# Attention, expert network and feed-forward network on one core: a reordered start, smaller weight transfers and an earlier seam

## The chip, the cores and the metric

The kernel runs on one core of a Trainium2 chip. A core has TensorE (PE, matrix products), VectorE (DVE), ScalarE (ACT), GpSimd (POOL) and SyncE (SP, which here only issues DMAs). PE writes to eight banks of PSUM; everything else lives in SBUF. The metric is the time of the device for one execution, in microseconds (us), lower is better; three executions were timed and one more was profiled.

## The reference, cut to what matters

```python
# 1. gated linear attention, B=4, H=8, S=768, D=48
for t in range(S):
    state = alpha[:, :, t, :, None] * state + einsum('bhd,bhe->bhde', k[:, :, t], v[:, :, t])
    y[:, :, t] = einsum('bhd,bhde->bhe', q[:, :, t], state)
x = y as 3072 rows of 384
# 2. first network: each row goes to the one expert (of 8) with the largest cosine
expert_idx = argmax(xn @ en.T / tau, axis=1); gate_w = its softmax probability
for e in range(E):
    h = maximum(x[mask] @ w1[e], 0)              # 384 -> 1024
    out[mask] = gate_w[mask, None] * (h @ w2[e]) # 1024 -> 384
# 3. second network, the same weights for all rows
h = x @ w_in                                     # 384 -> 2048
return maximum(0.01 * h, h) @ w_out              # 2048 -> 384
```

## The kernel before

**Stages.** The attention fills the first 120 us or so, and the routing (which row goes to which expert, a table of slots) the next 15. The first network then runs to about 441 us and the second to the end. All products have float32 operands cut into a high part (rounded by ACT to fp32r) and a low part (the rest, by DVE), and PE makes three products for each: high by high, high by low, low by high (`PARTS`). So each operand needs an ACT pass and then a DVE pass: `gx_round`/`gx_rest` for the gathered rows, `h_round`/`h_rest` for the hidden values, `split_hi`/`split_lo` for the weights, `y_round`/`y_rest` for the rows of the second network.

**First network.** Rows are sorted by expert into 31 blocks (`WINDOWS`) of 128 slots; block w uses buffers w & 1. POOL gathers a block's rows into `xg`; PE turns them (`turn_gx`, line 1484); ACT and DVE make `gxT`; PE computes the hidden values in two halves of 9 products (`block_hidden`, line 1508); ACT applies relu. Then the hidden values must be turned as well. For odd blocks, block 0 and block 30 PE does it (`turn_h`, line 1519) and `h_round` reads PSUM (line 815). For the other even blocks (`by_squares`) DVE turns 32 by 32 squares and SP moves the squares by 16 small DMAs (`hds<-hs`), and `h_round` reads those (line 819). DVE makes the low part (lines 1255 and 1258), and PE sums the second product over 24 products (`contract`, line 1528). DVE copies the sums to `ys` (line 1302), POOL scatters them to `y_rows`, which is in memory.

Each engine runs a `step(w, u)` for every block, in order of program, and its instructions wait on semaphores. In step w, PE does the hidden part of block w + 2, turns the rows of block w + 3, and then contracts block w. ACT does, in this order: `h_round(w)`, `relu(w + 2)` twice, `gx_round(w + 3)`, and where the block table says that a new expert follows (`follower`), `first_weights` for W1 or `second_weights` for W2. DVE has the matching order: `h_rest(w)`, its turn of block w + 2, `gx_rest(w + 3)`, small work, splits, copy of the sums. Only block 0's steps hold extra work: block 1's hidden part, the rows of block 2 turned after `turn_h(0, 0)`, and `place_slots`, 13 short DVE instructions (lines 1185 to 1212) that make `slot_dst`, the row to which each slot is scattered.

**Weights.** There are ten sets: eight experts, then `SET_IN` and `SET_OUT`, the second network's. A set has two halves (W1 and W2) of 12 KB a partition, 1536 KB in all. Memory delivers a half to `raw`; ACT writes the high part in three pieces, DVE the low part in three, into the set of `wts` with that parity. After DVE has read a half of `raw`, the next one may be loaded, and `load_half` is called right behind `split_hi` by the same engine, so ACT waits there for DVE (`w_lo`), then issues the DMA. ACT issues 16 of these, SP the first two (expert 1) and, before those, six smaller ones of 512 KB for expert 0 (`load_first`, line 489).

```python
def second_weights(w, e):
    act.wait_ge(ye_ready, w + 1)
    split_hi(act, e, next_set(act, e), W2_PIECES)
    load_half(act, 1, next_expert(act, e))
```

**Second network.** Six groups of 512 rows. For each of 16 slices of 128 hidden features, PE computes `inner` (9 products, line 1555) into one of two banks; ACT scales by 0.01 (`small`, line 909), DVE takes the maximum (`g`, line 1316), ACT and DVE make the parts of `gs` (912, 1318), and PE adds to the sums of four tiles (`outward`, line 1602, 12 products). `inner` runs two slices ahead. The first two slices of group 0 are computed in step 30, ahead of block 30's `contract`; before that, rows of group 0 are turned in step 29 (`y_turn`, `y_round`, `y_rest`). PE waits for `ys_ready` of block 30 before it goes on, since bank 6 is shared.

Of the kernel before, what the change touches and what calls it, by code (L numbers as in the profile page):

```python
# [24 lines left out]
def build(nc, qka, v, emb, tau, weights, x_dram, y_dram, gate_dram, out):  # L25
# [14 lines left out]
    WINDOWS = N // P + E - 1  # L40
# [34 lines left out]
    with ExitStack() as ctx:  # L75
# [328 lines left out]
        def split_hi(act, n, par, pieces):  # L404
            for j in pieces:
                if j % 3 == 0:
                    act.wait_ge(raw_in[j // 3], n * 16 + 48)
                cols = slice(j * PC, (j + 1) * PC)
                act.activation(set_of(par, 0, cols), raw[:, cols], ACT.Copy).then_inc(w_hi[j // 3], 1)  # L409

# [7 lines left out]
        def load_half(eng, half, n):  # L418

            eng.wait_ge(w_lo[half], n * 3)  # L420
            at = slice(half * 3 * PC, (half + 1) * 3 * PC)
            src = weights[n, half] if isinstance(n, int) else weights[ds(n, 1), half].rearrange("a p n -> (a p) n")
            eng.dma_start(raw[:, at], src, max_dma_last_dim=2048).then_inc(raw_in[half], 16)

        W1_PIECES, W2_PIECES = range(0, 3), range(3, 6)

# [279 lines left out]
        def _(act):  # L706
# [89 lines left out]
            def gx_round(w, u):  # L796
                act.wait_ge(gx_turned, w + 1)
                act.activation(gxT[:, u, 0], gxps, ACT.Copy).then_inc(gx_hi, 1)
# [41 lines left out]
            relu(0, 0, 1)  # L840
            act.wait_ge(tables_ready, 2)

            def y_round(t, u, k):
                act.wait_ge(yt_turned, t * KD + k + 1)
                act.activation(yT[:, 1 - u, 0, k], yf[:, (u * KD + k) % 2], ACT.Copy).then_inc(yt_hi, 1)

            def step(w, u):
                if isinstance(w, int) and w == 0:
                    for half in range(2):
                        relu(1, 1, half)  # L850
                    e, first = follower(act, 1)
                    with act.If(first > 0):
                        first_weights(0, 1)
                        first_weights(1, e)
                for half in range(2):
                    h_round(w, u, half)
                if isinstance(w, int) and w == 0:
                    gx_round(2, 0)
                    with act.If(act.snap(E - first) > 0):
                        first_weights(0, 1)  # L860
                if ahead(w, 2):
                    for half in range(2):
                        relu(w + 2, u, half)
                if ahead(w, 3):
                    gx_round(w + 3, 1 - u)
                if ahead(w, 2):
                    e, first = follower(act, w + 2)
                    with act.If(first > 0):
                        first_weights(w + 2, e)
                e, first = follower(act, w)  # L870
                with act.If(first > 0):
                    second_weights(w, e)
                if isinstance(w, int) and w == 1:
                    act.wait_ge(shift_done, 1)
                    act.activation(ex[:, :, :], lg[:, :, :], ACT.Exp).then_inc(exp_done, 1)
                if isinstance(w, int) and w == WINDOWS - 2:
                    for k in range(KD):
                        y_round(0, 0, k)
                if not ahead(w, 1):
                    split_hi(act, SET_OUT, 1, W1_PIECES)  # L880

            each_window(act, step)
# [19 lines left out]
            def groups(i, last):  # L902
                for u in range(2):
                    t = i * 2 + u
                    for f in range(FT):
                        s = t * FT + f
                        act.wait_ge(g_ready, s + 1)
                        act.wait_ge(g_done, s + 1)
                        act.activation(small[:, f % 2], gps[f % 2][:, :], ACT.Copy, scale=0.01).then_inc(small_done, 1)  # L909
                        act.wait_ge(g_done, s + 3)  # L910
                        act.wait_ge(l2_done, s + 1)
                        act.activation(gs[:, f % 4, 0], g[:, f % 2], ACT.Copy).then_inc(g_hi, 1)  # L912
                        if Y_FROM < f <= Y_FROM + KD and not (last and u == 1):
                            y_round(t + 1, 1 - u, f - Y_FROM - 1)
                        if f == 1 and t > 0:
                            for tt in range(TG):
                                o_copy(t - 1, 1 - u, tt)
                        if t == 0 and 2 <= f < 2 + len(W2_PIECES):
                            act.wait_ge(ye_ready, WINDOWS + 1)
                            split_hi(act, SET_OUT, 1, W2_PIECES[f - 2:f - 1])  # L920
# [7 lines left out]
        def _(dve):  # L928
# [237 lines left out]
            def y_turn(t, u, k):  # L1166

                if k == 0:
# [2 lines left out]
                dve.transpose(yf[:, (u * KD + k) % 2].rearrange("p (n r) -> p n r", r=SQ),  # L1171
                              yl[:, u, :, k * SQ:(k + 1) * SQ]).then_inc(yt_turned, 1)

            def y_rest(t, u, k):
                dve.wait_ge(yt_hi, t * KD + k + 1)
                dve.tensor_tensor(yT[:, 1 - u, 1, k], yf[:, (u * KD + k) % 2], yT[:, 1 - u, 0, k].bitcast(F32),
                                  ALU.subtract).then_inc(yt_lo, 1)
# [83 lines left out]
            def step(w, u):  # L1261
                if isinstance(w, int) and w == 0:
                    e, first = follower(dve, 1)
                    with dve.If(first > 0):
                        split_lo(dve, 1, 1, W1_PIECES)
                        split_lo(dve, e, next_set(dve, e), W1_PIECES)
                for half in range(2):
                    h_rest(w, u, half)
                if isinstance(w, int) and w == 0:
                    gx_rest(2, 0)  # L1270
                    with dve.If(dve.snap(E - first) > 0):
                        split_lo(dve, 1, 1, W1_PIECES)
                if ahead(w, 2) and by_squares(w + 2, u):
                    turn_h(w + 2, u)
                if ahead(w, 3):
                    gx_rest(w + 3, 1 - u)
                if isinstance(w, int) and w == 0:
                    place_slots()
                if isinstance(w, int) and w == 1:
                    shift_logits()  # L1280
                if isinstance(w, int) and w == 2:
                    make_gates()
                if ahead(w, 2):
                    e, first = follower(dve, w + 2)
                    with dve.If(first > 0):
                        split_lo(dve, e, next_set(dve, e), W1_PIECES)
                e, first = follower(dve, w)
                with dve.If(first > 0):
                    split_lo(dve, e, next_set(dve, e), W2_PIECES)
                if isinstance(w, int) and w == WINDOWS - 2:  # L1290
                    y_turn(0, 0, 0)
                    y_turn(0, 0, 1)
                    y_rest(0, 0, 0)
                    dve.wait_ge(yt_lo, 1)
                    y_turn(0, 0, 2)
                    y_rest(0, 0, 1)
                    y_rest(0, 0, 2)
                if not ahead(w, 1):
                    split_lo(dve, SET_OUT, 1, W1_PIECES)
                wait_scattered(dve, w, u, dve_turns)  # L1300
                dve.wait_ge(ye_ready, w + 2)
                dve.tensor_copy(ys[:, u, 0:D], yeps).then_inc(ys_ready, 1)  # L1302
# [1 line left out]
            each_window(dve, step, apart=2)  # L1304


            dve.sem_inc(g_done, 2)

            def groups(i, last):
                for u in range(2):  # L1310
                    t = i * 2 + u
                    for f in range(FT):
                        s = t * FT + f
                        dve.wait_ge(small_done, s + 1)

                        dve.tensor_tensor(g[:, f % 2], gps[f % 2][:, :], small[:, f % 2], ALU.max).then_inc(g_done, 1)  # L1316
                        dve.wait_ge(g_hi, s + 1)
                        dve.tensor_tensor(gs[:, f % 4, 1], g[:, f % 2], gs[:, f % 4, 0].bitcast(F32),  # L1318
                                          ALU.subtract).then_inc(g_lo, 1)
# [12 lines left out]
        def _(pe):  # L1332

            pe.sem_inc(ye_ready, 1)
            pe.sem_inc(l2_done, 4)
            pe.wait_ge(consts_made, MADE)

            def keep_busy(n, to, left, right):
# [232 lines left out]

            def step(w, u):
                if isinstance(w, int) and w == 0:
                    block_hidden(1, 1)
                if isinstance(w, int) and w == 0:
                    turn_h(0, 0)
                    turn_gx(2, 0)
                if ahead(w, 2):
                    block_hidden(w + 2, u, (lambda: turn_h(w, u)) if u == 1 else None)
                elif not by_squares(w, u):  # L1580
                    turn_h(w, u)
                if ahead(w, 3):
                    turn_gx(w + 3, 1 - u)
                if not ahead(w, 1):
                    pe.wait_ge(w_lo[0], SET_IN * 3 + 3)
                    pe.wait_ge(relu_done, WINDOWS * 2)
                    for f in range(2):
                        inner(0, 0, f)
                e = pe.snap(table(pe, w) & (E - 1))
                par = pe.snap(e & 1)  # L1590
                pe.wait_ge(w_lo[1], e * 3 + 3)
# [106 lines left out]
```

## Time and the profile before

| what | value |
|---|---|
| median of 3 runs | 845.28 us (842.88 to 846.42) |
| profiled execution | 847.34 us |
| its span, first to last instruction | 845.3 us |
| mean granted clock of PE | 0.992 |
| PE busy | 820.9 us, 97% |
| DVE, ACT, POOL busy | 434.2, 343.0, 203.4 us |

A busy share is of the span. PE takes a product of 128x512 in 0.23 us at full clock; its busy time is no proof of its peak rate. Where PE stands idle, the view of waits names the instruction that ended the idle time.

### The profile page before, as it was taken

How to read it: one execution, taken by the hardware profiler on the slowest of the kernel's cores; microseconds unless marked ns; L12 is line 12 of the kernel's file. 1: busy time of each engine (PE TensorE's matmuls, PEld its weight loads, DVE VectorE, ACT ScalarE, POOL GpSimd, SP SyncE). 2: the span in 40 equal slices, each digit the busy share in tenths (PEclk: the TensorE clock that was granted, in tenths of full speed). 3: DMA queues.
4: the chain of work that ended last, by engine and by line, in shares of the span. 5: the costliest groups of instructions: out<-in, count | busy, mean ns of one | idle time of the engine just before them, and what ended most of it. 6: DMA issues, size and time to landing. Idle time of an engine off the chain costs nothing.

```text
span 845.3 us, 17159 instructions
## 1 busy us (share of the span) xinstructions
PE 820.9 (97%) x5379; PEld 736.8 (87%) x5380; DVE 434.2 (51%) x672; ACT 343.0 (41%) x643; POOL 203.4 (24%) x279
## 2 busy tenths in 40 slices
PE   7999999799999999999989999999999999999998
PEld 7888887689889999889979998998998998998997
DVE  6899986664455465464355533533533433443332
ACT  3455564444444444453334323323323333333233
POOL 5666622033233223332214003003003001000100
PEclk8999999999999999999999999999999999999999
DMA  9987664545564447667113201201011000000101
GB/s 229 256 247 233 209 216 140 159 152 163 179 211 146 147 143 180 224 202 182 52 4 41 38 1 38 38 1 38 14 24 37 0 0 28 10 1 0 38 1 38
DMA packets 61719, 85.81 MB, mean 102 GB/s; under 512 B 26279, under 2 KB 40147, under 8 KB 61680
## 3 DMA queue, kind: packets, MB, share of 16 engines
q1 hardware_dynamic: 39952, 45.24, 20.1%
q10 hardware_dynamic: 15840, 25.23, 9.5%
q0 software_dynamic: 5888, 14.85, 5.2%
q8 instruction: 22, 0.36, 0.2%
q14 instruction: 17, 0.14, 0.1%
HBM read 63.69 MB, written 15.64 MB: 94 GB/s over the span
## 4 chain that ended last, share of the span: by engine, by line
PE 85%; DVE 5%; issue 3%; ACT 2%; ACTq 1%; DMA 1%; POOL 1%; DVEq 1%; SPq 0%; POOLq 0%
PE bank L1555 24%; PE bank L1602 24%; PE bank L1528 12%; PE bank L1508 12%; PE bank L1350 3%; PE bank L1390 2%; PE bank L1367 2%; DVE wts L415 1%; PE bank L1519 1%; PE bank L1356 1%; PE bank L1398 1%; ACT wts L409 1%; PE bank L1410 1%; DMA qkas<-qka 1%; ACTq L385 1%
## 5 line engine op out<-in xcount | busy, mean ns | idle before, releaser
L1555 PE MATMUL bank<-yT,wts 128*128 128x512 f32 x864 | 217.1, 395 | 1.6 <-DVE g L1316 1.6
L1602 PE MATMUL bank<-wts,gs 128*128 128x384 f32 x1152 | 215.4, 335 | 0.4 <-ACT os L900 0.2
L1602 PEld LDWEIGHTS bank<-wts,gs 128*128 128x128 f32 x1152 | 202.2, 188 | 10.6 <-issue 1.6
L1555 PEld LDWEIGHTS bank<-yT,wts 128*128 128x128 f32 x864 | 160.7, 188 | 32.6 <-DVE g L1316 1.9
L1316 DVE TENSOR_TENSOR g<-bank,small 128x512 f32<-128x512 f32 x96 | 66.4, 691 | 173.9 <-ACT small L909 173.9
L1528 PE MATMUL bank<-wts,hT 128*128 x744 | 138.6, 341 | 8.0 <-DVE hT L1255 4.2
L1508 PE MATMUL bank<-wts,gxT 128*128 (+1 forms) x549 | 136.2, 398 | 2.9 <-DVE gxT L1133 2.9
L1528 PEld LDWEIGHTS bank<-wts,hT 128*128 128x128 f32 x744 | 129.7, 190 | 10.0 <-issue 9.7
L909 ACT ACTIVATE small<-bank 128x512 f32<-128x512 f32 x96 | 57.6, 600 | 188.9 <-PE bank L1555 183.6
L1508 PEld LDWEIGHTS bank<-wts,gxT 128*128 128x128 f32 x549 | 102.6, 190 | 22.8 <-issue 3.1
L1318 DVE TENSOR_TENSOR gs<-g,gs 128x512 fp32r<-128x512 f32 x96 | 66.6, 694 | 67.0 <-ACT gs L912 67.0
L912 ACT ACTIVATE gs<-g 128x512 fp32r<-128x512 f32 x96 | 60.7, 632 | 73.0 <-DVE g L1316 73.0
L700 POOL DMA_INDIRECT out<-os,tokens x20 | 19.7, 985 | 288.1 <-ACT os L900 283.5
L415 DVE TENSOR_TENSOR wts<-raw,wts 128x1024 f32 (+1 forms) x60 | 70.2, 1220 | 22.9 <-ACT wts L409 20.0
L677 POOL DMA_INDIRECT y_rows<-ys,idst x31 | 32.3, 1042 | 177.8 <-DVE ys L1302 162.9
L409 ACT ACTIVATE wts<-raw 128x1024 f32 (+1 forms) x60 | 59.4, 1051 | 12.5 <-issue 12.4
L815 ACT ACTIVATE hT<-bank 128x512 fp32r<-128x512 f32 x34 | 18.5, 596 | 61.1 <-PE bank L1519 51.5
L1302 DVE COPY ys<-bank 128x384 f32<-128x384 f32 x31 | 17.2, 553 | 46.8 <-PE bank L1528 46.8
L819 ACT ACTIVATE hT<-hds 128x512 fp32r<-128x512 f32 x28 | 16.2, 625 | 60.3 <-DMA hds<-hs 40.7
L1255 DVE TENSOR_TENSOR hT<-bank,hT 128x512 fp32r<-128x512 f32 x34 | 21.9, 686 | 26.6 <-ACT hT L815 26.6
L651 POOL DMA_INDIRECT xg<-x_rows,isrc x27 | 29.6, 1096 | 23.8 <-POOL isrc L646 23.8
L604 POOL TENSOR_TENSOR qt<-qkas,decay 112x512 f32<-112x512 f32 x24 | 30.7, 1280 | 17.4 <-DVE decay L951 17.4
(174 smaller groups left out, 772.5 us busy)
## 6 DMA issues: line engine op xcount, KB each, us to landing
raw<-weights ACTq DMA_DIRECT2D x16, 1536.0 KB, 7.7
qkas<-qka SPq DMA_DIRECT2D x20, 675.5 KB, 4.9
hds<-hs SPq DMA_DIRECT2D x224, 32.0 KB
vs<-v SPq DMA_DIRECT2D x24, 192.0 KB, 3.9
x_rows<-xs SPq DMA_DIRECT2D x24, 192.0 KB, 3.7
yl<-y_rows SPq DMA_DIRECT2D x20, 192.0 KB, 5.0
raw<-weights SPq DMA_DIRECT2D x6, 512.0 KB, 5.3
raw<-weights SPq DMA_DIRECT2D x2, 1536.0 KB, 7.1
```

The costliest lines, as they stand in the source:

```text
L409: act.activation(set_of(par, 0, cols), raw[:, cols], ACT.Copy).then_inc(w_hi[j // 3], 1)
L415: dve.tensor_tensor(set_of(par, 1, cols), raw[:, cols], set_of(par, 0, cols).bitcast(F32), ALU.subtract).then_inc(w_lo[j // 3], 1)
L604: pool.tensor_tensor(qt[0:PW, b], q_in[b][0:PW], decay[0:PW, b], ALU.mult).then_inc(qt_ready, 1)
L677: pool.indirect_dma_start(out=y_dram, out_offset=bass.IndirectOffsetOnAxis(ap=idst[:, u:u + 1].bitcast(U32), axis=0), in_=ys[:, u, :], in_ ...
L909: act.activation(small[:, f % 2], gps[f % 2][:, :], ACT.Copy, scale=0.01).then_inc(small_done, 1)
L912: act.activation(gs[:, f % 4, 0], g[:, f % 2], ACT.Copy).then_inc(g_hi, 1)
L1316: dve.tensor_tensor(g[:, f % 2], gps[f % 2][:, :], small[:, f % 2], ALU.max).then_inc(g_done, 1)
L1318: dve.tensor_tensor(gs[:, f % 4, 1], g[:, f % 2], gs[:, f % 4, 0].bitcast(F32), ALU.subtract).then_inc(g_lo, 1)
L1508: m = pe.matmul(hps[u][half][:, :], gxT[:, u, x_part, k * P:(k + 1) * P], set_of(par, w_part, slice(n, n + HALF)), start=(k == 0 and (x_pa ...
L1528: m = pe.matmul(yeps, hT[:, h_part, k * P:(k + 1) * P], set_of(par, w_part, slice(n, n + D)), start=(k == 0 and (h_part, w_part) == (0, 0) ...
L1555: m = pe.matmul(gps[f % 2][:, :], wts[:, 0, w_part, n:n + P], yT[:, 1 - u, y_part, k], start=(k == 0 and (w_part, y_part) == (0, 0)), stop ...
L1602: m = pe.matmul(ops[tt], gs[:, f % 4, g_part, tt * P:(tt + 1) * P], wts[:, 1, w_part, f * D:(f + 1) * D], start=(f == 0 and (g_part, w_par ...
```

## The change


- `load_half` issues three DMAs of 1024 columns (4 KB a partition) where it issued one of 3072, each adding 16 to `raw_in`; `split_hi` waits for all three before its first piece.
- In step 0, PE turns the rows of block 2 between the two halves of block 1's hidden part and no longer behind `turn_h(0, 0)`. ACT does `gx_round(2, 0)` between the two relus of block 1, ahead of `h_round(0)`. DVE does `gx_rest(2, 0)` and `place_slots()` ahead of `h_rest(0)`; `place_slots` stood further down in that step.
- The turn of group 0's rows for the second network goes from step 29 to step 28.
- `inner(0, 0, 0)` goes from step 30 to step 29, ahead of block 29's `contract`; `inner(0, 0, 1)` stays in step 30. ACT makes `small` of slice 0, and DVE `g` of slice 0, in step 29, ahead of the split of `SET_OUT`'s W1, which goes from step 30 to step 29 too. The increment of `g_done` by 2 moves from DVE, behind its last step, to PE's start.

```diff
-                    act.wait_ge(raw_in[j // 3], n * 16 + 48)
+                    act.wait_ge(raw_in[j // 3], n * 48 + 48)
...
-            at = slice(half * 3 * PC, (half + 1) * 3 * PC)
-            eng.dma_start(raw[:, at], src, max_dma_last_dim=2048).then_inc(raw_in[half], 16)
+            for j in range(3):
+                eng.dma_start(raw[:, (half * 3 + j) * PC:(half * 3 + j + 1) * PC],
+                              src[:, j * PC:(j + 1) * PC]).then_inc(raw_in[half], 16)
...
+            def scale_small(s, f=0):
+                act.wait_ge(g_ready, s + 1)
+                act.wait_ge(g_done, s + 1)
+                act.activation(small[:, f % 2], gps[f % 2][:, :], ACT.Copy, scale=0.01).then_inc(small_done, 1)
...
                 if isinstance(w, int) and w == 0:
-                    for half in range(2):
-                        relu(1, 1, half)
+
                     e, first = follower(act, 1)
                     with act.If(first > 0):
                         first_weights(0, 1)
                         first_weights(1, e)
-                for half in range(2):
-                    h_round(w, u, half)
-                if isinstance(w, int) and w == 0:
+                    relu(1, 1, 0)
                     gx_round(2, 0)
+                    relu(1, 1, 1)
+                    h_round(0, 0, 0)
+                    h_round(0, 0, 1)
                     with act.If(act.snap(E - first) > 0):
                         first_weights(0, 1)
+                else:
+                    for half in range(2):
+                        h_round(w, u, half)
...
-                if isinstance(w, int) and w == WINDOWS - 2:
+                if isinstance(w, int) and w == WINDOWS - 3:
                     for k in range(KD):
                         y_round(0, 0, k)
-                if not ahead(w, 1):
+                if isinstance(w, int) and w == WINDOWS - 2:
+                    scale_small(0)
                     split_hi(act, SET_OUT, 1, W1_PIECES)
...
+            def leaky(s, f=0):
+                dve.wait_ge(small_done, s + 1)
+                dve.tensor_tensor(g[:, f % 2], gps[f % 2][:, :], small[:, f % 2], ALU.max).then_inc(g_done, 1)
...
+                    gx_rest(2, 0)
+                    place_slots()
                 for half in range(2):
                     h_rest(w, u, half)
                 if isinstance(w, int) and w == 0:
-                    gx_rest(2, 0)
                     with dve.If(dve.snap(E - first) > 0):
                         split_lo(dve, 1, 1, W1_PIECES)
...
-                if isinstance(w, int) and w == 0:
-                    place_slots()
...
-                if isinstance(w, int) and w == WINDOWS - 2:
+                if isinstance(w, int) and w == WINDOWS - 3:
                     y_turn(0, 0, 0)
...
-                if not ahead(w, 1):
+                if isinstance(w, int) and w == WINDOWS - 2:
+                    leaky(0)
                     split_lo(dve, SET_OUT, 1, W1_PIECES)
...
-            dve.sem_inc(g_done, 2)
...
+            pe.sem_inc(g_done, 2)
...
-                    block_hidden(1, 1)
-                if isinstance(w, int) and w == 0:
+                    block_hidden(1, 1, lambda: turn_gx(2, 0))
                     turn_h(0, 0)
-                    turn_gx(2, 0)
...
-                if not ahead(w, 1):
-                    pe.wait_ge(w_lo[0], SET_IN * 3 + 3)
-                    pe.wait_ge(relu_done, WINDOWS * 2)
-                    for f in range(2):
-                        inner(0, 0, f)
+                if isinstance(w, int) and w >= WINDOWS - 2:
+                    if w == WINDOWS - 2:
+                        pe.wait_ge(w_lo[0], SET_IN * 3 + 3)
+                        pe.wait_ge(relu_done, WINDOWS * 2)
+                    inner(0, 0, w - WINDOWS + 2)
```

## Rows read from the trace of the kernel before

**Rows 1.** The page, engines: busy us, share of span, instructions.

```profile
PE 820.9 (97%) x5379; PEld 736.8 (87%) x5380; DVE 434.2 (51%) x672; ACT 343.0 (41%) x643; POOL 203.4 (24%) x279
```

**Rows 2.** Stretches: length, busy time of PE, PEld, DVE, ACT, POOL, granted clock, DMA, GB/s.

```profile
150.00:157.50 7.50, 6.22 (x22) 4.99 (x23) 4.86 (x6) 3.38 (x5) 0.65 (x1) 0.77 0.43 126
...
168.00:176.00 8.00, 6.42 (x27) 6.33 (x28) 4.02 (x12) 4.40 (x8) 2.58 (x5) 0.79 0.74 247
```

**Rows 3.** Timeline, first blocks: start, us, engine, line, operation; in brackets idle time before.

```profile
138.94 1.01 POOL L651 DMA_INDIRECT xg<-x_rows,slot_src  x1 [2.04 <-PE bank L1477]
...
147.04 1.03 PE L1519 MATMUL bank<-ident,hs 128*128 128x128 f32 x8
...
151.28 5.99 PE L1508 MATMUL bank<-wts,gxT 128*128 x18 [2.88 <-DVE gxT L1133]
154.25 0.40 ACTq L423 DMA_DIRECT2D raw<-weights  x1
...
159.01 0.16 DVE L1185 TENSOR_SCALAR slot_val<-slot_val 128x31 f32<-128x31 f32 x1
...
163.79 3.50 DVE L415 TENSOR_TENSOR wts<-raw,wts 128x1024 f32 x3 [2.05 <-issue]
...
167.46 0.40 ACTq L423 DMA_DIRECT2D raw<-weights  x1
...
169.58 5.99 PE L1528 MATMUL bank<-wts,hT 128*128 x24 [2.48 <-DVE hT L1255]
```

**Rows 4.** Tile `xg`, the gather issued between 138.5 and 141 us.

```profile
DMA to landing us min/median/max: 6.5/6.5/6.5
```

**Rows 5.** Line 423: duration in ns (min/median/max), first and last start, landing.

```profile
L423 ACTq DMA_DIRECT2D raw<-weights x16: 389/397/429, 154.2 to 392.6; - x16
...
DMA to landing us min/median/max: 6.8/7.7/8.5
```

**Rows 6.** Timeline, DMAs issued back to back by SP and by ACT.

```profile
106.90 1.42 SPq L489 DMA_DIRECT2D raw<-weights  x3
...
435.13 1.17 ACTq L886 DMA_DIRECT2D token_gates<-gates  x2
```

**Rows 7.** Waits over the span: us in total, times, longest.

```profile
ACT hT L819 <- DMA hds<-hs: 40.7, 8, 5.6
...
PE bank L1528 <- DVE hT L1255: 4.2, 3, 2.5
PE bank L1528 <- DVE hT L1258: 3.8, 4, 1.0
```

**Rows 8.** Timeline, blocks 5, 6 and 25, each behind a load.

```profile
206.62 1.09 ACT L815 ACTIVATE hT<-bank 128x512 fp32r<-128x512 f32 x2 [2.79 <-PE bank L1519]
207.25 1.29 DVE L1255 TENSOR_TENSOR hT<-bank,hT 128x512 fp32r<-128x512 f32 x2 [0.85 <-ACT hT L815]
...
208.30 4.45 PE L1528 MATMUL bank<-wts,hT 128*128 x24
...
218.03 4.45 PE L1528 MATMUL bank<-wts,hT 128*128 x24 [0.82 <-DVE hT L1258]
...
393.70 1.29 DVE L1255 TENSOR_TENSOR hT<-bank,hT 128x512 fp32r<-128x512 f32 x2 [0.84 <-ACT hT L815]
...
394.80 4.43 PE L1528 MATMUL bank<-wts,hT 128*128 x24
```

**Rows 9.** Timeline, the seam between the networks.

```profile
427.85 4.48 PE L1528 MATMUL bank<-wts,hT 128*128 x24 [1.27 <-DVE hT L1255]
...
441.69 0.56 DVE L1302 COPY ys<-bank 128x384 f32<-128x384 f32 x1 [3.08 <-PE bank L1528]
...
443.20 2.37 PE L1555 MATMUL bank<-yT,wts 128*128 128x512 f32 x9 [1.62 <-DVE g L1316]
```

**Rows 10.** The chain that ended last: start, us, what.

```profile
437.40 4.19 PE bank L1528 x24
...
447.66 2.10 PE bank L1555 x9
```

More of the change, by code:

```diff
@@ L906, in groups @@
                         s = t * FT + f
-                        act.wait_ge(g_ready, s + 1)
-                        act.wait_ge(g_done, s + 1)
-                        act.activation(small[:, f % 2], gps[f % 2][:, :], ACT.Copy, scale=0.01).then_inc(small_done, 1)
+                        if not (isinstance(t, int) and t == 0 and f == 0):
+                            scale_small(s, f)
                         act.wait_ge(g_done, s + 3)
@@ L1313, in groups @@
                         s = t * FT + f
-                        dve.wait_ge(small_done, s + 1)
-                        dve.tensor_tensor(g[:, f % 2], gps[f % 2][:, :], small[:, f % 2], ALU.max).then_inc(g_done, 1)
+                        if not (isinstance(t, int) and t == 0 and f == 0):
+                            leaky(s, f)
                         dve.wait_ge(g_hi, s + 1)
```

## The prediction, made before the changed kernel was run

> **What bounds the kernel now.** I began with the page: TensorE (PE) is busy for 97% of the span, so only time in which PE stands still, or runs slow, can be won or lost [rows 1]. The granted clock by stretches comes next. It is full but for two stretches of the first network, 150 to 157.5 us at 0.77 and 168 to 176 at 0.79 [rows 2]. The timeline shows why: PE stood idle for 2.88 us and 2.48 us just before, and 18 and 24 products behind the gaps took 5.99 us each [rows 3], where 24 take 4.45 at full clock [rows 8]. The list of waits then tells what PE waits for in the blocks: seven waits for `hT` on the vector engine (DVE), 8.0 us [rows 7], and one for `gxT`, the 2.88 us. Two more sit at the seam between the networks, 1.27 us (one of those seven) and 1.62 us [rows 9]. From 446 us on PE never stops, and the change leaves that part alone. Weights land 6.8 to 8.5 us after their issue [rows 5], and the list of waits has none in which a split waits for `raw`: their landing bounds nothing.
>
> **Part 1, block 2 turned early and slots placed early.** Before, the order on the DVE after block 2 is: turn its rows, `gx_rest(3)`, `place_slots` from 159.01 to 161.74 (2.65 us behind `gx_rest`; the end is 2.05 before 163.79), 2.05 us of register work, three halves of W2's split from 163.79 to 167.29, and only then may ACT issue the load at 167.46 and make `hT` of block 1, which PE gets at 169.58 [rows 3]. That is 1.7 us from the end of the issue to PE.
> Now PE turns `gx` 2 between block 1's halves, at about 145.2 us. The gather for it, issued at 138.94, landed 6.5 us later, at 145.4 [rows 3, 4], so this costs some 0.3 us at most. ACT and DVE have `gxT` 2 ready at 147.1, PE is done with `turn_h(0)` at 148.7 (0.3 for the gather and 0.3 for three transposes behind 148.07 [rows 3]), and block 2 starts there, with no gap, for 151.28, and the clock stays up. PE is 4.4 us ahead when block 2 ends (152.85 for 157.27).
> It can't keep that. `place_slots` now stands before `h_rest(0)`, which ends at 151.1 instead of 150.2, so the split of expert 1's W1 ends 0.4 later and ACT's load goes out at 154.7. With three issues (below) ACT is free at 156.0. Two `relu` (1.1 us, as the pair of 1.09 in [rows 8]), the copy of `gx` 3 and its rest on the DVE take 2.35, to 158.35. Then 2.05 us of registers, 3.5 of splitting to 163.9, 1.45 for the load, 1.7 to PE: block 1's `contract` starts at 167.05, for 169.58. **Gain 2.5 us.** PE meanwhile waits twice: 1.6 us for `gxT` 3 (157.4 to 158.95) and 2.7 us before 167.05, so I let the clock fall there as before. Bounds: 1.3 us if the gather lands 1 us later behind three weight transfers, 4.3 us if the clock stays up (the 5.99 becomes 4.45, and some).
>
> **Part 2, three transfers a half.** One issue holds ACT's queue for 0.39 to 0.43 us, with 1536 KB in it [rows 5]; one with 512 KB holds SP's for 0.43, and three of them take 1.42 us [rows 6]. So the time goes with the number and not the bytes, and two more issues cost 0.9 us. Two small ones on ACT itself took 1.17 [rows 6], which bounds the price above at 1.2 us. Below nothing but zero bounds it. I take 0.9, the nearest row.
> What is queued behind? `load_half` is the last act of ACT's step, and the first of the next is `h_round`, which makes the `hT` PE needs for `contract`. In [rows 8] ACT issues until 206.51, starts `hT` at 206.62, DVE has the first half at 207.95 (207.25 and half of its 1.29, rounded up), and PE starts at 208.30, 0.35 behind, with no time to spare. ACT loads 14 more times after the two of part 1. Read like this, PE's slack behind each is: zero or already a wait in eight (blocks 3, 5, 6, 8, 15, 19, 20, 22), 0.02 in 17, 0.04 in 11, 0.05 in 25 (5, 6 and 25 are in [rows 8]), 0.11 in 13, 0.54 in 23 and 0.6 in 9. With 0.9 us more: 8 x 0.9 = 7.2, then 0.88, 0.86, 0.85, 0.79, 0.36 and 0.3, **loss 11.2 us**. The losses add up because each chain (turn, split, subtract, load) starts again from PE's own progress. At 1.2 us an issue pair it is 15.4; at 0.1 it is 1.0; at 0.43 it equals the gains of parts 1 and 3.
> The Trainium skill, "DMA: Bandwidth & Descriptors", section "Anatomy of one DMA — SWDGE (gpsimd) path", gives some 50 ns for the sequencer's dispatch of a DMA. By that two more would be 0.1 us and this part 1.0 us; the trace's 0.40 us for each issue, on another queue than that section's, disagrees.
> The data itself: weights now come in larger pieces beside `hds<-hs`. ACT waited 40.7 us in eight times for those moves [rows 7], but PE had 0.45 to 1.4 us to spare behind each in the timeline, so an earlier landing wins nothing, and one later by 1 us would cost at most 1.5 us in all. I take zero.
>
> **Part 3, the seam.** Now one `inner` piece stands before block 29's `contract` and one before block 30's. It takes 2.1 us (9 products [rows 10]) and covers the 1.27 us wait, whose `hT` is ready at 427.85, or 428.3 with the `y` turns now ahead of it on the DVE, against 428.7 when PE comes to it: gain 1.27 and 0.3 of slow start (4.48 [rows 9] for 4.19 [rows 10]). Before, `small` and `g` of piece 0 were made only when block 30's sums were copied, hence 1.62 us and a slow start of 0.27 (2.37 for 2.10) [rows 9, 10]. Now they are made in step 29, and PE waits only for the copy of the sums, 0.1 + 0.56 [rows 9] + 0.1 = 0.75 us. The split of W1 on DVE, in step 29 too, ends near 434.0, and the copy of block 29's sums and the first half of `hT` 30 at 435.25, 0.2 us before PE wants it: tight, but enough. **Gain 2.4 us**, 1.3 if that cover is short, 3.3 if the last copy is hidden as well.
>
> **The sum.** -2.5 + 11.2 - 2.4 = +6.3 us on an execution of 847.3 us, span 845.3. The median of the runs is 845.28, 2.1 below that execution, so I carry the difference over to it: **851.5 us**, slower by 0.7%.
>
> **Rivals.**
> 1. *The issues don't hold up PE* (other side). If ACT got rid of an issue in 0.05 us, as a queue that takes them in parallel would allow, only 1.0 us is lost: -2.5 + 1.0 - 2.4 = -3.9, 841.4 us. It decides where a pair of issues costs under 0.43 us. Against it stand all rows of an issue: none is under 0.39 [rows 5, 6]. With zero it is 840.4. Chance 0.13. The skill's 50 ns would give this case.
> 2. *The clock falls at the longer waits.* Behind loads for blocks 6, 8, 20 and 22 PE already waits 0.8 to 1.0 us [rows 8, 7]; these become 1.75 to 2.0. A gap of 1.62 was followed by no fall [rows 9, 10], one of 2.48 by one [rows 3]. If it falls at all four, each costs 5.99 - 4.45 = 1.54 more: 6.2, 857.7 us. Chance 0.22.
> 3. *ACT is stopped by its own descriptors.* Three transfers in a row could fill the queue so that an issue takes a microsecond or more. SP's three at 106.90 did not [rows 6]. With 1.0 us more for each of 14: 865 us. Chance 0.05.
> 4. *Smaller loss, larger gain*: the clock stays up in part 1 and some losses are absorbed by what waits anyway. +11.2 becomes 8, the gains 6.5: 846.8 us. Chance 0.15.
> The forecast itself: 0.45.
>
> **How the numbers follow.** Likeliest case alone: 848.5 to 855.5 (bounds of parts 1 and 3, and an issue pair between 0.75 and 1.1 us). The range takes rivals 2 and 4 in and leaves 1, 3 and their like out: **844 to 860 us**. About 0.5% is what a measurement of this kernel can tell from no change, so faster means below 841.1 and slower above 849.5. Faster: the half of rival 1 below that line and a little of large gains, 0.08. Same: the other half, rival 4 and the low end of the forecast, 0.2. Slower 0.72.
>
> **What would show it.** Right, if the row of the line that issues in `load_half` has 48 issues on ACT's queue of 0.4 us each and the three of a half span 1.3; if the list of waits has PE waiting for `hT` some 15 times and 18 us instead of seven and 8.0; if `contract` of block 1 starts near 167; if an inner piece stands before each of the last two `contract` with no gap around it, and 0.75 us behind the last. Wrong in part 2, if `hT` follows the first issue by 0.1 us, or if an issue takes under 0.2. Wrong in part 1, if PE waits for `xg` over 1 us at 145 or the two stretches of low clock are gone. Wrong in part 3, if PE waits over 0.5 us for `hT` in block 30. Rival 2 shows as more stretches with a granted clock under 0.9.

## The result, and the profile after

The changed kernel took 852.74 us (851.99 to 853.10, four runs), the kernel before 844.33 in the same comparison: ratio 1.0096, 95% interval 1.0071 to 1.0122. The change costs about 1%, and the forecast of 851.5 us, slower, held. The profiled execution took 852.63 us with a span of 850.9.

To see where the time went, I cut both spans at the same four instructions: the first product of block 0, the second products (`contract`) of blocks 1 and 28, and the first `outward` product of the second network. The kernel before has its `contract` of block 1 in [rows 3] (169.58); its other three, by the timeline of PE:

```profile
138.39 2.30 PE L1499 MATMUL bank<-wts,gxT 128*128 128x512 f32 x9 [0.24 <-ACT gxT L836]
...
421.35 4.35 PE L1528 MATMUL bank<-wts,hT 128*128 x24
...
445.41 2.25 PE L1602 MATMUL bank<-wts,gs 128*128 128x384 f32 x12
```

The changed kernel, same view, with the start's steps and the seam (lines have moved by some ten):

```profile
137.08 2.32 PE L1510 MATMUL bank<-wts,gxT 128*128 128x512 f32 x9 [0.24 <-ACT gxT L837]
...
146.91 4.36 PE L1519 MATMUL bank<-wts,gxT 128*128 x18
...
152.83 1.32 ACTq L423 DMA_DIRECT2D raw<-weights  x3
154.20 1.09 ACT L810 ACTIVATE hr<-bank 128x512 f32<-128x512 f32 x2 [3.46 <-issue]
...
157.11 2.35 PE L1519 MATMUL bank<-wts,gxT 128*128 x9 [1.32 <-DVE gxT L1142]
...
161.66 1.39 ACTq L423 DMA_DIRECT2D raw<-weights  x3
...
163.10 1.08 ACT L816 ACTIVATE hT<-bank 128x512 fp32r<-128x512 f32 x2 [4.04 <-issue]
...
164.77 5.97 PE L1539 MATMUL bank<-wts,hT 128*128 x24 [2.05 <-DVE hT L1268]
...
429.23 4.35 PE L1539 MATMUL bank<-wts,hT 128*128 x24
...
434.21 2.36 PE L1566 MATMUL bank<-yT,wts 128*128 128x512 f32 x9
...
436.41 4.33 PE L1539 MATMUL bank<-wts,hT 128*128 x24
...
448.80 2.36 PE L1566 MATMUL bank<-yT,wts 128*128 128x512 f32 x9 [0.91 <-DVE ys L1315]
...
450.99 2.27 PE L1611 MATMUL bank<-wts,gs 128*128 128x384 f32 x12
```

| stage | before | after | difference |
|---|---|---|---|
| to block 0's first product | 138.39 | 137.08 | -1.3 |
| to block 1's `contract` ("start") | 31.19 | 27.69 | -3.5 |
| to block 28's `contract` ("blocks") | 251.77 | 264.46 | +12.7 |
| to the first `outward` ("seam") | 24.06 | 21.76 | -2.3 |
| to the end | 399.89 | 399.91 | 0 |

The first row is not the change's: in the 14 profiled executions (one for each kernel below) that point lay between 134.9 and 138.4, with nothing changed ahead of it but an increment of a semaphore on PE. In the start the gap of 2.88 us before block 2 is gone (146.91 follows `turn_h` at once, and 18 products take 4.36 us for 5.99). A wait of 1.32 for `gxT` 3 and one of 2.05 for block 1 are left. In the seam blocks 29 and 30 no longer wait, and 0.91 us is left behind the last sums. The loss is all in the blocks. The list of waits:

```profile
PE bank L1539 <- DVE hT L1268: 8.7, 7, 2.1
PE bank L1539 <- DVE hT L1271: 6.7, 4, 2.1
...
PE bank L1539 <- issue: 1.4, 3, 0.6
```

That is 11 waits and 15.4 us for `hT` (8.7 and 6.7), or 14 and 16.8 with the three that show no releaser ("issue"), where [rows 7] had seven and 8.0. The line that issues, and block 5 as in [rows 8]:

```profile
L423 ACTq DMA_DIRECT2D raw<-weights x48: 339/358/567, 152.8 to 400.4; - x48
```

```profile
202.62 1.54 ACTq L423 DMA_DIRECT2D raw<-weights  x3
204.28 1.08 ACT L816 ACTIVATE hT<-bank 128x512 fp32r<-128x512 f32 x2 [3.90 <-issue]
...
204.91 1.29 DVE L1268 TENSOR_TENSOR hT<-bank,hT 128x512 fp32r<-128x512 f32 x2 [1.99 <-ACT hT L816]
...
205.99 1.33 PE L1539 MATMUL bank<-wts,hT 128*128 x6 [1.08 <-DVE hT L1268]
```

Three issues hold the queue for 1.54 us; ACT's `hT` follows 0.12 later, DVE and PE in their turn, and PE, which had no wait in this block before, stands for 1.08 us.

### The profile page after: what moved, and what is told of

The parts are those of the page before. It is cut to its first block, busy times and chain, and to the rows that moved or that the text cites. A ratio compares the mean times of both kernels' runs of the same rounds, so it can differ in the third digit from the quotient of the medians.

```text
span 850.9 us, 17254 instructions
## 1 busy us (share of the span) xinstructions
PE 819.3 (96%) x5379; PEld 734.0 (86%) x5380; DVE 434.1 (51%) x672; ACT 341.9 (40%) x643; POOL 200.0 (24%) x279
## 4 chain that ended last, share of the span: by engine, by line
PE 80%; DVE 5%; issue 5%; ACTq 3%; ACT 3%; DMA 1%; POOL 1%; DVEq 0%; SPq 0%; POOLq 0%
PE bank L1566 24%; PE bank L1611 24%; PE bank L1539 11%; PE bank L1519 9%; PE bank L1361 2%; PE bank L1401 2%; DVE wts L415 2%; PE bank L1378 2%; ACT wts L409 2%; ACTq L423 2%; PE bank L1409 1%; PE bank L1367 1%; PE bank L1530 1%; ACTq L385 1%; PE bank L1421 1%
## 5 line engine op out<-in xcount | busy, mean ns | idle before, releaser
L1539 PE MATMUL bank<-wts,hT 128*128 x744 | 138.5, 341 | 17.0 <-DVE hT L1268 8.7
L1519 PE MATMUL bank<-wts,gxT 128*128 (+1 forms) x549 | 134.9, 395 | 1.3 <-DVE gxT L1142 1.3
L409 ACT ACTIVATE wts<-raw 128x1024 f32 (+1 forms) x60 | 59.5, 1055 | 11.2 <-issue 10.8
L652 POOL DMA_INDIRECT xg<-x_rows,isrc x27 | 29.6, 1095 | 23.8 <-POOL isrc L647 23.8
```

The lines of the kernel that those rows point to most:

```text
L1519: m = pe.matmul(hps[u][half][:, :], gxT[:, u, x_part, k * P:(k + 1) * P], set_of(par, w_part, slice(n, n + HALF)), start=(k == 0 and (x_pa ...
L1539: m = pe.matmul(yeps, hT[:, h_part, k * P:(k + 1) * P], set_of(par, w_part, slice(n, n + D)), start=(k == 0 and (h_part, w_part) == (0, 0) ...
```

## Experiments

Stages below are read from PE's timeline at the same four instructions; ratios are to the kernel before, timed anew beside each group of runs (its medians were 844.1 to 844.3 us, 843.3 beside E12). A stage comes from one profiled execution. Where PE's clock fell in it, it is some 1.5 us longer; that is so in the blocks of the kernel before, the changed one, E3, E6, E8 and E9, and in the starts of the kernel before and of E2.

| kernel | median, us | ratio (95%) | start | blocks | seam |
|---|---|---|---|---|---|
| before | 844.3 | | 31.2 | 251.8 | 24.1 |
| changed | 852.7 | 1.0096 (1.0071 to 1.0122) | 27.7 | 264.5 | 21.8 |
| E1 one transfer | 837.4 | 0.9910 (0.9885 to 0.9936) | 25.9 | 251.0 | 21.8 |
| E2 three transfers alone | 858.7 | 1.0177 (1.0142 to 1.0212) | 32.3 | 263.0 | 24.0 |
| E3 one big, two tiny | 855.4 | 1.0135 (1.0104 to 1.0166) | 28.3 | 265.5 | 21.8 |
| E4 two transfers | 842.0 | 0.9977 (0.9963 to 0.9992) | 26.8 | 255.9 | 21.8 |
| E5 start alone | 838.0 | 0.9920 (0.9899 to 0.9941) | 25.9 | 251.1 | 24.0 |
| E6 slots late | 840.4 | 0.9944 (0.9923 to 0.9965) | 29.6 | 251.7 | 21.8 |
| E7 one, late | 842.8 | 0.9983 (0.9965 to 1.0002) | 25.2 | 255.8 | 21.8 |
| E8 three, late | 849.0 | 1.0047 (1.0028 to 1.0066) | 25.8 | 262.9 | 22.0 |
| E9 one, behind | 841.7 | 0.9969 (0.9950 to 0.9989) | 25.1 | 258.0 | 21.8 |
| E10 three, behind | 843.4 | 0.9986 (0.9965 to 1.0007) | 25.8 | 256.1 | 21.8 |
| E11 turn late | 838.0 | 0.9922 (0.9890 to 0.9954) | 26.2 | 250.2 | 21.8 |
| E12 seam alone | 841.9 | 0.9983 (0.9968 to 0.9998) | 29.5 | 250.4 | 21.8 |

### E1 to E4: the count of issues or the data

**E1.** The changed kernel with `load_half` and its wait as before.

```diff
-            for j in range(3):
-                eng.dma_start(raw[:, (half * 3 + j) * PC:...], src[:, j * PC:...]).then_inc(raw_in[half], 16)
+            eng.dma_start(raw[:, at], src, max_dma_last_dim=2048).then_inc(raw_in[half], 16)
```

> The changed kernel with one transfer a half again, the new start and the new seam kept. Theory A (two more issues on ScalarE's queue ahead of the hidden values cost 12.7 us between block 1's and block 28's second product, as the two traces differ): 12 to 13 us under the changed kernel's 852.7, so 838.5 to 841 us, about 0.6% faster than before; TensorE waits for hT behind loads as before, 0.5 to 1.0 us in five blocks and none in the others. Rival B (the loss comes from the new start or seam, which leave ScalarE later than before in all later blocks): stays within 2 us of 852.7.

837.4 us, 0.9% faster than before and 15.4 under the changed kernel, more than the 12 to 13 that I expected: 13.5 in the blocks and 1.8 in the start. Of the 13.5, 1.0 is in the step behind block 1's `contract`, whose products ran slow in the changed kernel (5.97 us) and not in E1 (4.42). Rival B is out. Its list of waits and block 5:

```profile
PE bank L1538 <- DVE hT L1270: 4.1, 5, 1.0
...
PE bank L1538 <- DVE hT L1267: 1.8, 2, 1.0
```

```profile
198.54 0.40 ACTq L423 DMA_DIRECT2D raw<-weights  x1
199.05 1.09 ACT L815 ACTIVATE hT<-bank 128x512 fp32r<-128x512 f32 x2 [2.72 <-PE bank L1529]
```

**E2.** The kernel before, with only the edit of `load_half` and `n * 48 + 48`.

> The kernel before with three transfers a half and nothing else. Theory A: 844.3 plus 12.7 plus one more pair of issues ahead of block 1 (0.9 to 1.3), so 857 to 859 us, 1.6% slower. Rival B: little or nothing, under 847 us, since the start and the seam are as they were.

858.7 us, as theory A has it. The blocks lose 11.3 us and the start 1.1. Block 1's products ran slow in the kernel before (5.99 us) and not in E2 (4.43), so the issues take 12.8 of the blocks: the loss doesn't need the new start or seam.

**E3.** Three transfers of 2944, 64 and 64 columns, cut into pieces of 2 KB at most as before.

```diff
+            for lo, hi in ((0, 3 * PC - 128), (3 * PC - 128, 3 * PC - 64), (3 * PC - 64, 3 * PC)):
+                eng.dma_start(raw[:, half * 3 * PC + lo:half * 3 * PC + hi], src[:, lo:hi], max_dma_last_dim=2048).then_inc(raw_in[half], 16)
```

> The changed kernel, three transfers a half of unequal size: 2944 columns cut as before into pieces of 2 KB, then 64 and 64 columns. The count of issues is that of the changed kernel, the data nearly that of one transfer. Theory A (the count of issues): 852 to 854 us, the three issues of a half span 1.3 us on ScalarE's queue. Rival C (the larger pieces of 4 KB or the three transfers' data hold up the moves hds<-hs and the gathers): as with one transfer, 838.5 to 841 us.

855.4 us, 1.4 over the upper end of theory A, and the three issues span 1.50 to 1.68 us and not 1.3. Two issues of 32 KB cost no less than two of 512 KB; rival C is out. The issues and the timeline of block 5:

```profile
L423 ACTq DMA_DIRECT2D raw<-weights x48: 339/407/610, 150.9 to 400.1; - x48
```

```profile
200.05 1.00 ACTq L423 DMA_DIRECT2D raw<-weights  x2
201.17 1.08 ACT L815 ACTIVATE hT<-bank 128x512 fp32r<-128x512 f32 x2 [3.97 <-issue]
...
202.88 3.40 PE L1538 MATMUL bank<-wts,hT 128*128 x18 [1.13 <-DVE hT L1267]
```

(The x2 are the last two of three.)

**E4.** Two transfers, 2048 and 1024 columns, `n * 32 + 48`.

> The changed kernel with two transfers a half, 2048 and 1024 columns. Theory A: one more issue and not two, so half of 12.7 us is gone, less what the slack in six blocks takes: 845 to 847 us. Rival C (pieces): pieces are as large as with three, 852 us. A rival within A, that the first extra issue costs nothing and the queue fills with the second: 840 us.

842.0 us, 10.8 under the changed kernel and 4.6 over one transfer: less than half of the 15.4, and better than the 845 to 847 I gave. By stages the first extra issue costs 4.9 us in the blocks, the second 8.6, or some 7.1 without the slow products of block 1 in the changed kernel. Block 5 shows the first at 0.46 us (0.86 for 0.40), so PE waits 0.40:

```profile
198.24 0.86 ACTq L423 DMA_DIRECT2D raw<-weights  x2
199.21 1.09 ACT L815 ACTIVATE hT<-bank 128x512 fp32r<-128x512 f32 x2 [3.26 <-issue]
...
200.92 2.37 PE L1538 MATMUL bank<-wts,hT 128*128 x12 [0.40 <-DVE hT L1267]
```

Over the 16 loads two issues hold the queue for 0.84 to 1.09 us, three for 1.32 to 1.73. Load by load the second extra issue adds 0.55 us on average, about what the first does (0.52). It costs more in the blocks because the first has used up the slack: from block 8 to 9 E4 takes 9.56 us, the changed kernel 9.94, the kernel before 9.55.

### E5, E6, E11, E12: the parts of the gain

**E5.** E1 with the seam of the kernel before.

> Only the new start (block 2 turned and slots placed sooner), one transfer a half, the seam as before. If the three parts add up, the seam's 2.3 us come back and nothing else: 839.5 to 840 us (one transfer with both parts had 837.4), the stage from first product to block 1's second product stays near 25.9 us for 31.2 before. Rival: the two parts help each other through the order on ScalarE, then 837.4 or over 841.

The stages add up as expected: start 25.9, seam 24.0. The median, 838.0, is under the 839.5 to 840 that I expected and only 0.65 us over E1's, while the seams differ by 2.3. The two profiled executions differ by 1.25 us, since E5's came to block 0's first product 1.2 us sooner; why the medians agree so closely is not shown.

**E6.** E1, with `place_slots()` behind `gx_rest(3)` as before.

```diff
                     gx_rest(2, 0)
-                    place_slots()
...
                     gx_rest(w + 3, 1 - u)
+                if isinstance(w, int) and w == 0:
+                    place_slots()
```

> One transfer a half, new start and seam, but place_slots back at its old place behind the turn of block 2's squares. Theory A (the vector engine's 2.7 us of place_slots stood ahead of the W2 split on which ScalarE's load and then block 1's hT wait): block 1's second product comes 2 to 3 us later, 839.5 to 841 us. Rival D (the gain of the start is the early turn of block 2 alone, which feeds TensorE): under 838.3 us.

840.4 us, start 29.6: the early slots are worth 3.7 us of the start in the trace, more than the 2 to 3 that I expected, and 3.0 in the median. PE waits 4.35 us before block 1's `contract` here, against 1.02 in E1.

**E11.** E1, with block 2 turned behind `turn_h(0, 0)` again (PE, ACT and DVE), slots early.

```diff
-                    block_hidden(1, 1, lambda: turn_gx(2, 0))
+                    block_hidden(1, 1)
                     turn_h(0, 0)
+                    turn_gx(2, 0)
```

> One transfer a half, new seam, slots placed early, but block 2 turned behind turn_h of block 0 as before. With slots late the start took 29.6 us, with both early 25.9, with both late 31.2. If the early turn is worth the rest, the start takes 27 to 28 us and the total 839 to 840 us; if the slots alone bring the gain, 837.4.

838.0 us, start 26.2. The early turn is worth 0.4 us in the start, which a measurement can't tell from nothing. It only moves PE's wait from ahead of block 2 to behind it: in E11 PE waits 2.24 us before block 2 and not at all before block 1's `contract`, in E1 only there, 1.02 us. What sets block 1's `hT` is DVE's order (E6).

**E12.** The kernel before with the new seam alone.

> The kernel before with the new seam alone. If the parts add up, the stage from block 28's second product to the first of the second network's outward products takes 21.8 us for 24.1, and the stages ahead of it stay at 31.2 and 251.8: 842 us, 0.27% faster. Rival: what the seam wins is given back in the second network, whose ScalarE and VectorE work of slice 0 is now done early: 844.

841.9 us, seam 21.8. The median is 1.4 us under the 843.3 of the kernel before beside it, and the ratio's interval just leaves 1 out. Its start took 29.5 us with the code of the kernel before, which took 31.2; why is told under the hardware.

### E7 to E10: the same issues at another place in the queue

**E7, E8.** From step 1 on, ACT issues a load one step later, behind `h_round`, after it has read the block table twice more; one and three transfers.

```diff
+            def late_loads(w):
+                if ahead(w, 1):
+                    e, first = follower(act, w + 1)
+                    with act.If(first > 0):
+                        load_half(act, 0, next_expert(act, e))
+                e, first = follower(act, w - 1)
+                with act.If(first > 0):
+                    load_half(act, 1, next_expert(act, e))
...
                     for half in range(2):
                         h_round(w, u, half)
+                    late_loads(w)
```

> One transfer a half, and from step 1 on ScalarE issues it in the next step, behind that step's h_round, at the price of two more table reads a step on its sequencer. Theory A (what counts is that an issue, and the wait for the split before it, stand ahead of the hidden values): the waits of 0.8 to 1.0 us in blocks 3, 6, 8, 20 and 22 go, 4.6 us and 0.28 of slow start for each, so 831 to 833 us. Rival E (hT waits for the vector engine's split, which stands ahead of h_rest anyway): at most 1 us below 837.4.

> The same with three transfers a half. Theory A: the place in the queue decides and not the count, so within 2.5 us of the kernel with one late transfer (the first two loads of the start are still in their old place and cost 1 to 2 us): 832 to 835 us. Rival C (the three transfers' data or their use of the shared descriptor path hurts): 845 us or more.

Both missed: 842.8 and 849.0 us, 10 to 17 more than expected. The waits of blocks 3, 8 and 22 are gone, new ones stand in blocks 4, 12, 14, 16 and 18, and block 2's has grown from 0.30 us in E1 to 1.60. The reads and the load now stand ahead of the relus, whose result the moves `hds<-hs` carry to the even blocks. For E7, list of waits:

```profile
PE bank L1548 <- DVE hT L1280: 7.1, 8, 1.6
...
ACT hT L819 <- DMA hds<-hs: 58.0, 11, 6.6
```

ACT's waits for the moves were 40.7 us before [rows 7] and 45.5 in E1. Here the count matters again, 7.1 us in the blocks between E7 and E8, some 5.5 without a fall of the clock in E8. Three issues delay the relus further: in E7 the relu behind the load issued at 293.35 us starts 0.54 us after the start of that issue and has waited for PE; in E8 the relu behind the same load, issued from 298.19 us on, starts 1.56 us after it, 0.11 behind the third issue. E8's 849.0 also lies where rival C put it; that the data cost nothing here was not tested by itself, but E10 below moves the same data without the loss.

**E9, E10.** The table reads ahead of `h_round`, the load behind both relus and `gx_round` of the next step.

```diff
+                    pending = due_loads(w)
                     for half in range(2):
                         h_round(w, u, half)
...
                     gx_round(w + 3, 1 - u)
+                if not (isinstance(w, int) and w == 0):
+                    late_loads(pending)
```

> One transfer a half. From step 1 on ScalarE reads the tables of the pending load ahead of h_round, where it waits for TensorE or the moves anyway, and issues the load in the next step behind h_round, both relus and gx_round. Theory A: in the kernel with one late transfer the table reads and the load stood ahead of the relus, so the moves hds<-hs of the even blocks began later; here nothing urgent stands behind a load, so the waits of blocks 3, 6, 8, 20 and 22 go and no new ones come in the even blocks: 831 to 834 us. Rival E (the vector engine's own split sets hT): 836 to 838 us.

> The same with three transfers a half. Theory A (place in the queue, not count): within 3 us of the kernel with one transfer so placed, the start's two loads (1.8 us) included, 833 to 837 us. If three transfers cost through the data path: 842 us or more.

841.7 and 843.4 us. E9 misses by 8 us and lies above the range of its rival, 836 to 838, too. E10's 843.4 lies in the range for a cost through the data path, 842 or more, but E9 with one transfer is nearly there as well, and the difference decides: E10's blocks take 256.1 us against 258.0 for E9, 256.4 without a fall of the clock in E9. So with the issues behind the urgent work, three cost no more than one in the blocks: that part of the theory holds. The medians are 1.7 us apart, 0.8 of it in the start, whose loads were not moved. With one transfer the new place is worse than the old one (E9 4.3 us over E1, E7 5.4), with three it is better (E10 9.3 us under the changed kernel, E8 3.8). Only one wait of PE for `hT` is left, and ten short ones of another kind have come; list of waits of E9, and its chain at block 6:

```profile
PE bank L1553 <- DVE hT L1285: 1.3, 1, 1.3
...
PE bank L1553 <- issue: 5.7, 10, 0.7
```

```profile
209.35 0.55 PE bank L1509 x3
209.90 0.71 issue
210.60 4.43 PE bank L1553 x24
```

In seven of the ten PE stands 0.63 to 0.74 us between the turn of the next rows and `contract` and waits for nothing that the profile shows. Which step of its own queue that is, I didn't test.

## Why the prediction was right

**Part 2, the step that decides.** Its mechanism is shown: issues cost by their number (E1, E3, E4), wherever `hT` or a relu is queued behind them (E8 over E7), and nothing where neither is (E10 against E9). The size was 11.2 us and came to 12.7 between the two traces, 12.8 and 12.5 in E2 and E1 once block 1's slow products are taken out. The pair of issues was put at 0.9 us and took 0.9 to 1.3. The other term I left out is PE's slow start behind a new wait: from block 10 to 11 the kernel takes 10.71 us for 9.51 in E1, with a wait of 0.97. I had charged these 0.25 us at the seam and not here, where eight blocks got a wait that they hadn't. The list of the 14 blocks held: new waits in 5, 9, 11, 13, 15, 17, 19 and 25, longer ones in 3, 6, 8, 20 and 22. In 23 the timeline marks no wait, but from block 22 to 23 the kernel takes 9.92 us for 9.55, the 0.36 that I expected. The sizes held less well. From one `contract` to the next, blocks 3, 5, 11, 15, 19 and 25 lost 1.1 to 1.3 us and 8 and 22 1.0, where I had 0.85 to 0.9. Blocks 6 and 20 lost only 0.5 and 0.35 where I had 0.9 each: my statement that each chain starts again from PE's own progress, so that the losses add up, does not hold for these two, and why was not tested. So the total of 11.2 is nearer to the truth than its terms are.

**Part 1.** Sized 2.5, measured 3.5 us. The order of the steps is as forecast. Two pieces were short: the wait for `gxT` 3 was 1.3 and not 1.6 us, and DVE stood 1.41 us before W2's split where I carried over 2.05. ACT began its part of that split 0.45 us behind `gxT` 3, for 1.18 before; why the gap shrank was not tested. The 3.5 also leans on the trace of the kernel before, whose clock had fallen at block 2: E12 has the same code in the start, kept its clock behind the same gap and took 29.5 us, and against that the gain is 1.8. My sum took the execution with the fall as its baseline and so counted the end of the fall as won by closing the gap. The three transfers take 1.8 us of what the start could win (E1: 5.3). My text credited the turn and the slots together; with one transfer, E6 and E11 show that nearly all of it is the slots.

**Part 3.** Sized 2.4, measured 2.3; what is left behind the last sums is 0.91 for 0.75.

**The rivals.** The issues do hold up PE, so rival 1 falls: no issue on ACT's queue took under 0.34 us, those of 32 KB in E3 included. The 50 ns that the Trainium skill, "DMA: Bandwidth & Descriptors", section "Anatomy of one DMA — SWDGE (gpsimd) path", has for a dispatch is of another queue, and as a price for an issue on ACT's these traces disagree with it. Rival 2 did not come in the profiled execution: the waits of blocks 8 and 22 grew to 2.06 and 2.04 us and left the clock at 1.00, and those of blocks 6 and 20 reached only 1.28 where it had 1.75. It is not refuted, though: in E3, with as many issues, a wait of 2.24 in block 22 was followed by a fall (below). Rival 3 did not come: none of 48 issues took over 0.57 us.

**The sum.** 6.3 us on the profiled execution came to 5.3 there (847.34 to 852.63) and 8.4 between the medians; the two measures differ by 3.1, and runs of the kernel before spread by 3.5, 842.9 to 846.4. The mechanism was right, but that 851.5 came within 1.2 us of 852.74 is in part luck: part 2 was 1.5 us too small, part 1 took 1.0 more off in the trace, and a single fall of the clock more or less moves the difference by 1.5.

## What to carry to other kernels

Count DMA issues by what is queued behind them on the issuing engine, not by their bytes: one more cost 0.34 to 0.69 us here, and where the next instruction feeds the bounding engine with no slack, nearly every pass with a load pays it, here with some 0.2 us of slow start on top. Split a transfer only if somebody waits for its first part; here the consumer waited for all three, and none of the waits was for the data. Before moving an issue, ask which of the next step's instructions it will stand in front of instead: with one transfer both of my placements were slower than the one at the end of the step, and with three both were faster. Of the kernels tried, the changed one with one transfer a half has the lowest median, 837.4 us, 0.9% under the kernel before; E5 and E11 are within 0.7 us of it.

## What the runs showed of the hardware

**The clock's fall doesn't follow from the length of the gap alone.** The start of E12 has the code and the gaps of [rows 3], 2.79 and 2.45 us, but its products behind them take 4.36 and 4.45 us and not 5.99. Timeline and stretches (columns as in [rows 2]) of E12:

```profile
150.43 4.36 PE L1519 MATMUL bank<-wts,gxT 128*128 x18 [2.79 <-DVE gxT L1141]
...
167.12 4.45 PE L1539 MATMUL bank<-wts,hT 128*128 x24 [2.45 <-DVE hT L1267]
```

```profile
148.00:156.00 8.00, 5.57 (x27) 4.82 (x28) 6.50 (x8) 5.40 (x9) 1.03 (x1) 1.00 0.44 143
...
166.00:174.00 8.00, 6.88 (x36) 6.42 (x37) 5.33 (x14) 4.93 (x10) 2.82 (x6) 1.00 0.77 255
```

In the changed kernel a gap of 2.05 us before block 1 was followed by a fall and one of 2.04 before block 22 by none:

```profile
160.00:170.00 10.00, 7.95 (x37) 7.30 (x35) 5.57 (x14) 4.09 (x7) 2.78 (x5) 0.83 0.73 233
...
371.00:376.00 5.00, 2.96 (x18) 2.72 (x17) 3.34 (x6) 4.25 (x7) 2.99 (x5) 1.00 0.96 342
```

The other runs have more of both. A fall stood behind waits of 1.33 us (E9, block 2, with one of 0.85 shortly before), 1.81 (E8, block 24), 2.24 (E3, block 22) and 4.35 (E6, block 1). None stood behind 2.24 (E3, block 8, in the same execution), 2.36 (E3, block 1) and 3.63 (E2, block 1). Timeline of E9, E3 and E2:

```profile
171.50 6.01 PE L1553 MATMUL bank<-wts,hT 128*128 x24 [1.33 <-DVE hT L1285]
...
371.67 6.00 PE L1538 MATMUL bank<-wts,hT 128*128 x24 [2.24 <-DVE hT L1270]
...
168.64 4.43 PE L1529 MATMUL bank<-wts,hT 128*128 x24 [3.63 <-DVE hT L1256]
```

So a fall costs 1.5 to 1.7 us and comes or not with the execution, and two of them are much of the spread of 3.5 us between runs of the kernel before. In its 20 executions beside E9 to E11, the six with a mean granted clock of 0.992 took 847.1 to 847.8 us and the five at 0.998 or 1.000 took 841.9 to 843.7. What decides it beyond the gap, these runs leave open.

**An issue's price on ACT's queue goes by the number and not by the bytes.** The kernel before takes 0.39 to 0.43 us for one issue of 1536 KB, E4 0.84 to 1.09 for two, the changed kernel 1.32 to 1.73 for three of 512 KB, and E3 1.50 to 1.68 for one of 1472 KB and two of 32 KB. Whether ACT's queue or what takes its issues sets the price, and why some loads are dearer than others, was not tried.
